# Queries and keys of a head transposed together, copied out whole, split by GpSimd in place and spread over the partitions by four DMAs

## The chip, the cores and the metric

The kernel runs on one core of one Trainium2 chip. The metric is the device time of one execution in microseconds (us), from first to last instruction with a little around it; the profile also gives the span alone.

## What is computed

Three layers in a row: attention in which a query sees only keys of its own cluster, a top-1 mixture of eight experts, and a feed-forward layer. Only the attention is touched by the change.

```python
# q, k, v: (2, 8, 768, 64) float32; centroids: (8, 16, 64)
q_assign = np.argmax(einsum('bhsd,hcd->bhsc', q_n, c_n), axis=-1)   # nearest centroid
k_assign = np.argmax(einsum('bhsd,hcd->bhsc', k_n, c_n), axis=-1)
mask = q_assign[:, :, :, None] == k_assign[:, :, None, :]
scores = np.where(mask, scale * np.matmul(q, k.transpose(0, 1, 3, 2)), -1e9)
attn = softmax(scores);  attn_out = np.matmul(attn, v)
```

## The kernel before

The attention is a loop over 16 (batch, head) pairs, called heads here; the engines' programs are written out by hand and tied by semaphores. A head has six tiles of 128 positions. All big products are made from float32 numbers split in a high part (rounded to the matmul's format, fp32r) and a low part (the rest): a product is high x high plus the cross terms.

Head h is worked on in `attend(h)`, in six steps s = 0..5 on every engine. In a step, TensorE (PE) transposes probabilities (`transpose_probs`, L1245, six transposes), makes the scores of one query tile (`scores`, L1231/L1232, tiles 4 and 5 of head h in s = 0, 1, then tiles 0 to 3 of head h+1), and adds to the output (`prob_values`, L1259/L1261). ScalarE (ACT) copies the transposed probabilities out of PSUM (L629), takes the exponential (`expo`, L603) of the scores whose row maximum VectorE (DVE) has made (`rowmax`, L871); DVE makes the low half of the probabilities (L923). `transpose_probs` at s = 0 and s = 3 waits for the exponentials of three tiles (`exp_done`): at s = 3 the last is that of tile 5, which ACT makes in s = 2. `outputs_back` (L1273, in s = 1 and 4) waits for `o_t`, which ACT copies (L612).

The operands of head h+2 are prepared in between, through one PSUM bank (number 7):

- GpSimd (POOL), `split_operands` (L419, L421): each [128 x 64] tile of q and k becomes [high | low], 128 wide, in `halves`; it runs a head further ahead.
- PE, `operands` (L1185): twelve transposes of `halves` tiles per head, in four batches of three, at s = 0, 2, 3 and 4 (the last one split: one transpose before `outputs_back`, two after). A batch waits for bank 7.
- The batch is copied out by ACT (`copy_operand`, L584) at s = 0, 3 and 4, and by DVE (`copy_second_batch`, L866) at s = 2; queries are scaled by 1/8 on the way.
- `cluster_scores` (L1196, s = 5) multiplies by the centroids, ACT copies `ct_sb` (L598), `cluster_rows` (L1205) brings the scores back to rows, DVE finds the clusters, and in s = 1 of `attend(h+1)` PE transposes their one-hot codes (`onehots`, L1214), which ACT (`copy_onehot`, L592, three copies, in s = 1) and DVE (L859) put beside the operands as extra rows that carry the mask.
- POOL's `copy_queries` (L445) and two DMAs on SP's queue (`move_keys`, L336 then L338, the second after the first has landed) put halves on the other 64 partitions. `scores(h+2, 0)`, in s = 2 of `attend(h+1)`, waits for all of it.

POOL also makes low halves of the first expert's weights in pieces (`split_piece`, L404) in heads 2 to 5 and 8 to 11. At the start the operands of heads 0 and 1 are made outside the loop; `warm` matmuls (L1166) fill PE's waits. At the end of the attention `attend(14)` has no operands to prepare (`ahead` is 1) and `attend(15)` nothing ahead.

In the row names below, `ps` is PSUM, `p_t` the transposed probabilities, `qk_t` the operands of the scores.

Of the kernel before, what the change touches and what calls it, by code (L numbers as in the profile page):

```python
# [26 lines left out]
F32 = mybir.dt.float32  # L27
# [8 lines left out]
P = 128  # L36
# [30 lines left out]
BATCH_OF = {0: 0, 2: 1, 3: 2, 4: 3}  # L67
FIRST_BANKS = ((4, 5, 6, 7), (4, 5, 6, 4))
# [6 lines left out]
WARM = (11, 11, 9)  # L75
# [6 lines left out]
def build(nc, q, k, v, centroids, w_gate, w_ogate, w1, w2, w_in, w_out, out):  # L82
# [58 lines left out]
    raw = place("raw", [P, 2, 2 * QT, D], F32, early)  # L141
    halves = place("halves", [P, 2 * QT, 2 * D], F32R, early)
# [5 lines left out]
    cen_t = place("cen_t", [P, 2, P], F32R, early)  # L148
# [15 lines left out]
    cst = place("cst", [P, 2, 14 * NC], F32R, small)  # L164
# [51 lines left out]
    with ctx:  # L216
# [16 lines left out]
        high_done, halves_done, tr_done, opa_done = sem("high_done"), sem("halves_done"), sem("tr_done"), sem("opa_done")  # L233
        keys_low, keys_high = sem("keys_low"), sem("keys_high")
        b2_done, vs_done, vhi_done = sem("b2_done"), sem("vs_done"), sem("vhi_done")
# [67 lines left out]
        def _(sp):  # L303
            sp.dma_start(cen[:, 0, :], centroids.rearrange("h c d -> (h c) d")).then_inc(cen_in, 16)

            def load_head(h, u):

                if h >= 2:
                    sp.wait_ge(halves_done, 2 * (h - 1))
                sp.dma_start(raw[:, u, 0:QT, :], q_h[bass.ds(h, 1)].squeeze(0)).then_inc(qk_in[u], 16)  # L310
                sp.dma_start(raw[:, u, QT:, :], k_h[bass.ds(h, 1)].squeeze(0)).then_inc(qk_in[u], 16)
# [20 lines left out]
            def move_keys(h):  # L332

                u = h % 2
                sp.wait_ge(ct_done, h + 1)
                sp.dma_start(qk_t[0:D, u, B2:B2 + QT, :].bitcast(F32), qk_t[D:, u, B1:B1 + QT, :].bitcast(F32)).then_inc(keys_low, 16)  # L336
                sp.wait_ge(keys_low, 16 * (h + 1))
                sp.dma_start(qk_t[D:, u, B1:B1 + QT, :].bitcast(F32), qk_t[0:D, u, B1:B1 + QT, :].bitcast(F32)).then_inc(keys_high, 16)  # L338

            move_keys(0)  # L340
            for h in range(2, BH):
                load_head(h, h % 2)
                move_keys(h - 1)
# [5 lines left out]
            move_keys(BH - 1)  # L349
# [14 lines left out]
        def _(pool):  # L364
# [15 lines left out]
            pool.tensor_copy(const_f[:], const_i[:]).then_inc(const_pool, 1)  # L380

# [30 lines left out]
            def split_operands(h, j, i, u, first):  # L412

                if j == 0:
                    pool.wait_ge(qk_in[u], 32 * (i + 1))
                if not first:
                    pool.wait_ge(tr_done, 4 * (h - 1) + 2 * (j + 1))
                t = slice(j * QT, (j + 1) * QT)
                pool.tensor_copy(halves[:, t, 0:D], raw[:, u, t]).then_inc(high_done, 1)  # L419
                pool.wait_ge(high_done, 2 * h + j + 1)  # L420
                pool.tensor_tensor(halves[:, t, D:], raw[:, u, t], halves[:, t, 0:D].bitcast(F32),  # L421
                                   ALU.subtract).then_inc(halves_done, 1)
# [11 lines left out]
            def place_centroids(h, u):  # L434
# [33 lines left out]
            def attend(h, i, u):  # L468
# [11 lines left out]
                if h + 3 < BH:  # L480
                    split_operands(h + 3, 0, i + 1 + u, 1 - u, False)
# [4 lines left out]
                if h + 2 < BH:  # L486
                    copy_queries(h + 2, u)
                if 2 * h < SPREAD:
                    spread(h, 0)
                if h + 3 < BH:  # L490
                    split_operands(h + 3, 1, i + 1 + u, 1 - u, False)
# [3 lines left out]
            split_operands(0, 0, 0, 0, True)  # L495
            split_operands(0, 1, 0, 0, True)
            pool.wait_ge(cen_ev, 2)
            place_centroids(0, 0)
            split_operands(1, 0, 0, 1, False)
            copy_queries(0, 0)  # L500
            split_operands(1, 1, 0, 1, False)
            pool.wait_ge(const_pool, 11)
            candidates(0)
            place_centroids(1, 1)
            split_values(0, 0, 0, True)
            copy_queries(1, 1)
            split_operands(2, 0, 1, 0, False)
            split_operands(2, 1, 1, 0, False)
# [64 lines left out]
        def _(act):  # L573
# [4 lines left out]
            def copy_operand(h, b, u, first, bank=7):  # L578

                if not first and b < 2:  # L580
                    act.wait_ge(s_done, QT * (h - 2) + HALF * (b + 1))
                act.wait_ge(tr_done, 4 * h + b + 1)
                t = (A1, B1)[b // 2] + HALF * (b % 2)
                act.activation(qk_t[:, u, t:t + HALF, :].rearrange("p t n -> p (t n)"), x_bank[bank], ACT.Copy,  # L584
                               scale=QSCALE if b < 2 else 1.0).then_inc(opa_done, 1)
# [28 lines left out]
            def attend(h, u, first, ahead):  # L614
                un = 1 - u
                for s in range(QT):
                    n = QT * h + s
                    if s == 3 and ahead >= 2:
                        copy_operand(h + 2, BATCH_OF[s], u, False)
# [10 lines left out]
                    if s in (0, 4) and ahead >= 2:  # L630
                        copy_operand(h + 2, BATCH_OF[s], u, False)
# [11 lines left out]
            for b in range(4):  # L643
                copy_operand(0, b, 0, True, FIRST_BANKS[0][b])
            copy_cluster_scores(0)
            for b in range(2):
                copy_operand(1, b, 1, True, FIRST_BANKS[1][b])
# [3 lines left out]
            copy_operand(1, 2, 1, True, FIRST_BANKS[1][2])  # L651
            expo(0, 1, 0)
            copy_operand(1, 3, 1, True, FIRST_BANKS[1][3])
# [135 lines left out]
        def _(dve):  # L789
            dve.memset(onehot[:], 0.0)  # L790
            dve.memset(qk_t[D:D + NC, :, A2:A2 + QT, :].bitcast(F32), 0.0)
            dve.memset(cen_s[:, 3, :].bitcast(F32), 0.0)
# [24 lines left out]
            dve.tensor_tensor(cen_s[:, 2, :], cen_u[:], cen_s[:, 0, :].bitcast(F32), ALU.subtract)\  # L817
                .then_inc(cen_d, 1)
            dve.memset(cst[:].bitcast(F32), 0.0).then_inc(cen_ev, 1)
            dve.wait_ge(cen_tr, 1)  # L820
            dve.tensor_copy(cen_t[:].rearrange("p j n -> p (j n)"), ps[:, 6, 0:2 * P]).then_inc(cen_ev, 1)
# [31 lines left out]
            def clusters(h):  # L853
                for step in (highest_score, best_clusters, highest_label, one_hot):
                    step(h)

# [4 lines left out]

            def copy_second_batch(h, u):
                dve.wait_ge(s_done, QT * (h - 2) + 2 * HALF)
                dve.wait_ge(tr_done, 4 * h + 2)
                t = A1 + HALF
# [684 lines left out]
```

## Time and profile before

| | |
|---|---|
| median of 3 runs | 839.55 us (839.29 to 839.87) |
| the profiled execution | 839.41 us |
| its span | 837.6 us |
| mean granted TensorE clock | 0.985 |
| PE busy | 801.6 us (96%) |
| DVE / ACT / POOL busy | 450.6 / 383.2 / 348.0 us |
| DMA queue of SP (q1) | 60.92 MB, 22.5% of 16 engines |

A matmul's end is modelled and matmuls overlap, so the distance between the starts of two rows tells what a group took, not the sum of durations. A row gives start and duration in us, the engine, the line, the operation, what it writes and reads, and in brackets the idle time of the engine before it and what ended that.

### The profile page before, as it was taken

How to read it: one execution, taken by the hardware profiler on the slowest of the kernel's cores; microseconds unless marked ns; L12 is line 12 of the kernel's file. 1: busy time of each engine (PE TensorE's matmuls, PEld its weight loads, DVE VectorE, ACT ScalarE, POOL GpSimd, SP SyncE). 2: the span in 40 equal slices, each digit the busy share in tenths (PEclk: the TensorE clock that was granted, in tenths of full speed). 3: DMA queues.
4: the chain of work that ended last, by engine and by line, in shares of the span. 5: the costliest groups of instructions: out<-in, count | busy, mean ns of one | idle time of the engine just before them, and what ended most of it. 6: DMA issues, size and time to landing. Idle time of an engine off the chain costs nothing.

```text
span 837.6 us, 13745 instructions
## 1 busy us (share of the span) xinstructions
PE 801.6 (96%) x4370; PEld 677.3 (81%) x4371; DVE 450.6 (54%) x795; ACT 383.2 (46%) x757; POOL 348.0 (42%) x343
## 2 busy tenths in 40 slices
PE   7999999999999949999999999989999999999994
PEld 4898999999999727888888888868888888888883
DVE  5788888888888865221221221234455444554442
ACT  4788888888788744222322322212222322332222
POOL 7345654455632028778767767764000100010001
PEclk9999999999999969999999999999999999999998
DMA  4344333423121148699669669682000100010001
GB/s 108 108 123 162 98 116 88 125 57 122 47 61 23 57 154 278 223 336 382 204 241 359 215 241 348 230 287 83 1 1 1 50 1 1 0 51 1 1 0 51
DMA packets 45429, 105.44 MB, mean 126 GB/s; under 512 B 5200, under 2 KB 12880, under 8 KB 44368
## 3 DMA queue, kind: packets, MB, share of 16 engines
q1 hardware_dynamic: 29584, 60.92, 22.5%
q0 software_dynamic: 15808, 44.04, 15.6%
q8 instruction: 21, 0.34, 0.2%
q14 instruction: 16, 0.13, 0.0%
HBM read 92.37 MB, written 6.29 MB: 118 GB/s over the span
## 4 chain that ended last, share of the span: by engine, by line
PE 89%; DVE 3%; ACT 2%; DMA 2%; issue 1%; POOL 1%; DVEq 0%; ACTq 0%; POOLq 0%
PE ps L1493 15%; PE ps L1480 15%; PE ps L1440 13%; PE ps L1420 11%; PE ps L1245 7%; PE ps L1261 4%; PE ps L1231 4%; PE ps L1232 4%; PE ps L1259 4%; PE ps L1273 2%; PE ps L1185 2%; PE ps L1430 2%; DMA raw_w<-in_moe_w 2%; PE ps L1205 2%; PE ps L1196 1%
## 5 line engine op out<-in xcount | busy, mean ns | idle before, releaser
L394 POOL TENSOR_TENSOR weights<-raw_w,weights 128x2048 fp32r<-128x2048 f32 x34 | 157.1, 4622 | 49.2 <-DMA weights<-in_moe_w 35.3
L1493 PE MATMUL ps<-weights,g_t 128*128 128x512 f32 x576 | 141.2, 394 | 2.5 <-DVE g_t L1151 2.5
L1480 PE MATMUL ps<-y_t,weights 128*128 128x512 f32 x576 | 139.3, 391 | 0.0
L1493 PEld LDWEIGHTS ps<-weights,g_t 128*128 128x128 f32 x576 | 107.3, 188 | 27.3 <-DVE g_t L1151 4.1
L1480 PEld LDWEIGHTS ps<-y_t,weights 128*128 128x128 f32 x576 | 108.1, 188 | 23.8
L923 DVE TENSOR_TENSOR p_t<-ps,p_t 128x384 fp32r<-128x384 f32 x192 | 98.9, 550 | 27.4 <-ACT p_t L629 27.0
L1420 PE MATMUL ps<-weights,x_t 128*128 x456 | 111.1, 399 | 1.7 <-DVE x_t L1084 1.7
L1440 PE MATMUL ps<-weights,h_t 128*128 x456 | 109.6, 396 | 2.3 <-issue 1.7
L565 POOL DMA_INDIRECT out<-y_sb,order_u x12 | 11.8, 979 | 240.3 <-ACT y_sb L776 238.4
L760 ACT ACTIVATE ps<-g_a,half 128x512 f32<-128x512 f32 x48 | 33.2, 692 | 149.7 <-DVE g_b L1146 149.7
L1420 PEld LDWEIGHTS ps<-weights,x_t 128*128 128x128 f32 x456 | 85.2, 190 | 20.0 <-issue 2.4
L1440 PEld LDWEIGHTS ps<-weights,h_t 128*128 128x128 f32 x456 | 84.3, 188 | 20.3 <-issue 2.8
L629 ACT ACTIVATE p_t<-ps 128x384 fp32r<-128x384 f32 x192 | 83.7, 490 | 24.4 <-PE ps L1245 24.0
L871 DVE TENSOR_REDUCE nmax<-ps 128x1 f32<-128x768 f32 x96 | 91.0, 949 | 4.9 <-PE ps L1232 3.3
L603 ACT ACTIVATE prob<-ps,nmax 128x768 f32<-128x768 f32 x96 | 87.2, 908 | 1.3 <-DVE nmax L871 0.9
L1245 PE MATMUL ps<-ident,prob 128*128 128x128 f32 x576 | 79.2, 273 | 1.3 <-ACT prob L603 0.8
L1231 PE MATMUL ps<-qk_t 128*128 128x384 f32 x192 | 73.2, 381 | 1.1 <-ACT prob L603 1.1
L1245 PEld LDWEIGHTS ps<-ident,prob 128*128 128x128 f32 x576 | 66.4, 140 | 5.0 <-ACT prob L603 1.8
L1261 PE MATMUL ps<-p_t,v_s 128*128 128x384 f32 x192 | 67.1, 350 | 1.1 <-DVE x_sb L897 0.6
L1232 PE MATMUL ps<-qk_t 80*128 80x384 f32 x192 | 65.1, 339 | 0.0
L714 ACT ACTIVATE h_t<-ps 128x1024 fp32r<-128x1024 f32 x19 | 19.5, 1025 | 92.3 <-PE ps L1430 92.3
L1145 DVE TENSOR_SCALAR g_a<-ps 128x512 f32<-128x512 f32 x48 | 33.1, 689 | 49.7 <-PE ps L1480 49.6
(178 smaller groups left out, 1076.4 us busy)
## 6 DMA issues: line engine op xcount, KB each, us to landing
raw_w<-in_moe_w SPq DMA_DIRECT2D x32, 1024.0 KB, 6.2
weights<-in_moe_w POOLq DMA_DIRECT2D x28, 1024.0 KB, 9.1
qk_t<-qk_t SPq DMA_DIRECT2D x32, 192.0 KB, 2.6
raw_w<-in_moe_w_in SPq DMA_DIRECT2D x4, 1024.0 KB, 6.0
weights<-in_moe_w_in POOLq DMA_DIRECT2D x4, 1024.0 KB, 7.8
raw_w<-in_moe_w_out SPq DMA_DIRECT2D x4, 1024.0 KB, 7.9
weights<-in_moe_w_out POOLq DMA_DIRECT2D x4, 1024.0 KB, 12.7
raw<-in_q SPq DMA_DIRECT2D x16, 192.0 KB, 2.9
```

The lines of the kernel that those rows point to most:

```text
L394: pool.tensor_tensor(weights[:, unit % 2, 1, c * CHUNK:(c + 1) * CHUNK], low_chunk(unit, c), high_chunk(unit, c).bitcast(F32), ALU.subtrac ...
L603: act.activation(prob[:, c, :].rearrange("p (a n) -> p a n", a=2), s_ps[c % 2], ACT.Exp, bias=nmax[:, c % 2:c % 2 + 1], accum_out=sums[:, ...
L871: dve.tensor_reduce(nmax[:, c % 2:c % 2 + 1], s_ps[c % 2], AX.XY, ALU.max, negate=True)\
L923: dve.tensor_tensor(p_t[:, s % 2, 1, t], pt_ps[:, t], p_t[:, s % 2, 0, t].bitcast(F32), ALU.subtract).then_inc(ptl_done, 1)
L1231: mm(o, qk_t[:, u, A1 + c, :], b1, start=True, stop=False)
L1232: last = mm(o, qk_t[0:D + NC, u, A2 + c, :], b2, start=False, stop=True)
L1245: last = tr(ps[:, 4 + t, c * P:(c + 1) * P], prob[:, HALF * g + c, k:k + P], ident[:])
L1261: last = mm(ot_ps, v_s[:, u, k, :], p_t[:, s % 2, 0, t, :], start=(k == 0), stop=(k == QT - 1))
L1420: last = mm(ps[:, n, :], x_t[:, u, a, k, :], flat[:, bass.ds(base + (b * UNIT + w), BANK)], start=(k == 0 and j == 0), stop=(k == KC - 1 a ...
L1440: last = mm(ps[:, 5 + u, :], h_t[:, a, n, :], flat[:, bass.ds(base + (b * UNIT + w), DM)], start=(n == 0 and j == 0), stop=(n == FC - 1 an ...
L1480: last = mm(ps[:, 4 + n % 2, :], wi[:, a, k, f * P:(f + 1) * P], y_ts[g % 2][:, b, k, :], start=(k == 0 and j == 0), stop=(k == KC - 1 and ...
L1493: last = mm(ps[:, t, :], g_t[:, n % 2, a, t * P:(t + 1) * P], wo[:, b, f, :], start=(f == 0 and j == 0), stop=(f == FC2 - 1 and j == 2))
```

## The change

`raw` holds q and k of a tile side by side, [128 x (64 | 64)], loaded so by the two DMAs (runs of 64 numbers instead of 384). PE transposes it unsplit: six transposes per head in two batches, at s = 0 and s = 2. The result, queries on partitions 0 to 63 and keys on 64 to 127, is copied out whole by ACT (`copy_whole`) with a scale per partition (1/8 or 1, the new tile `qscale`). POOL makes the high and the low half from that copy in place in `qk_t` (`split_operands`, after the transposes now). Four DMAs per head place the halves on the other partitions (`place_halves`). DVE's copy at s = 2 and POOL's `copy_queries` are gone, ACT's copies at s = 3 and 4 too, one at s = 2 is new. `copy_onehot` also waits for `k_low`. The centroids' table `cen_t` and `cst` are laid out for the new order (as many matmuls as before). At the start ACT makes the high half and DVE the low half out of PSUM, and the `warm` counts differ.

```diff
-BATCH_OF = {0: 0, 2: 1, 3: 2, 4: 3}
+BATCH_AT = {0: 0, 2: 1}
-WARM = (11, 11, 9)
+WARM = (5, 3, 11, 9)
...
# SP
-                    sp.wait_ge(halves_done, 2 * (h - 1))
-                sp.dma_start(raw[:, u, 0:QT, :], q_h[...])...
-                sp.dma_start(raw[:, u, QT:, :], k_h[...])...
+                    sp.wait_ge(tr_done, 2 * (h - 1))
+                sp.dma_start(raw[:, u, :, 0:D], q_h[...])...
+                sp.dma_start(raw[:, u, :, D:], k_h[...])...
...
+            def place_halves(h):
+                sp.wait_ge(high_done, 2 * (h + 1))
+                sp.dma_start(qk_t[0:D, u, A1:A1 + 2 * QT, :]..., high[0:D]...broadcast_to([D, 2, QT, P])).then_inc(q_high, 16)
+                sp.wait_ge(low_done, 2 * (h + 1))
+                sp.dma_start(qk_t[D:, u, A1:A1 + QT, :]..., low[0:D]).then_inc(q_low, 16)
                 sp.wait_ge(ct_done, h + 1)
+                sp.wait_ge(q_low, 16 * (h + 1))
+                sp.dma_start(low[0:D], low[D:]).then_inc(k_low, 16)
+                sp.wait_ge(q_high, 16 * (h + 1))
+                sp.dma_start(high[0:D], high[D:]).then_inc(k_high, 16)
...
# POOL
+            def split_operands(h, b, u):
+                if b == 0:
+                    pool.wait_ge(s_done, QT * (h - 1))
+                pool.wait_ge(whole_done, 2 * (h - 2) + b + 1)
+                pool.tensor_copy(hi, whole[:, b]).then_inc(high_done, 1)
+                pool.wait_ge(high_done, 2 * h + b + 1)
+                pool.tensor_tensor(lo, whole[:, b], hi.bitcast(F32), ALU.subtract).then_inc(low_done, 1)
...
# ACT
+            def copy_whole(h, b):
+                act.wait_ge(low_done, 2 * (h - 1) + b + 1)
+                act.wait_ge(tr_done, 2 * h + b + 1)
+                act.activation(whole[:, b], x_ps, ACT.Copy, scale=qscale[:, 0:1]).then_inc(whole_done, 1)
 
             def copy_onehot(h, j, u):
                 act.wait_ge(oh_tr, h + 1)
+                act.wait_ge(k_low, 16 * (h + 1))
...
-                    if s == 3 and ahead >= 2:
-                        copy_operand(h + 2, BATCH_OF[s], u, False)
+                    if s == 2 and ahead >= 2:
+                        copy_whole(h + 2, BATCH_AT[s])
...
# DVE
-                    if s == 2 and ahead >= 2:
-                        copy_second_batch(h + 2, u)
...
# PE
+                if b == 0:
+                    pe.wait_ge(qk_in[u], 32 * (i + 1))
+                for n in range(HALF):
+                    last = tr(x_bank[bank][:, n * P:(n + 1) * P], raw[:, u, HALF * b + n, :], ident[:])
...
-                    if s in (2, 3) and ahead >= 2:
-                        operands(h + 2, BATCH_OF[s], ...)
+                        operands(h + 2, BATCH_AT[s], i + 1, u, (oh_done, 2 * h + 4))
...
                     if s == 4:
-                        if ahead >= 2:
-                            operands(h + 2, 3, (opa_done, 4 * h + 11), (0,))
                         outputs_back(2 * h, h, u, first)
-                        if ahead >= 2:
-                            operands(h + 2, 3, None, (1, 2))
```

How ACT's instructions stood before, inside the loop, from the exponential of step 1 to the copy out of bank 7 in step 3:

```order
L603 ACTIVATE prob,sums<-ps,nmax 128x768 [waits max_done]
L626 ISA
L629 ACTIVATE p_t<-ps 128x384 [waits pv_done,pt_done]
L626 REGISTER_ALU
L629 ACTIVATE p_t<-ps 128x384 [waits pt_done]
L602 REGISTER_ALU
L603 ACTIVATE prob,sums<-ps,nmax 128x768 [waits max_done]
L582 REGISTER_ALU
L584 ACTIVATE qk_t<-ps 128x384 [waits tr_done]
```

How they stand there now, from the exponential of step 1 to that of step 2:

```order
L600 ACTIVATE prob,sums<-ps,nmax 128x768 [waits max_done]
L579 REGISTER_ALU
L580 REGISTER_ALU [waits low_done]
L581 ACTIVATE whole<-ps,qscale 128x384 [waits tr_done]
L623 ISA
L626 ACTIVATE p_t<-ps 128x384 [waits pv_done,pt_done]
L623 REGISTER_ALU
L626 ACTIVATE p_t<-ps 128x384 [waits pt_done]
L599 REGISTER_ALU
L600 ACTIVATE prob,sums<-ps,nmax 128x768 [waits max_done]
```

The copy out of bank 7 stood behind the exponential of step 2; now it stands ahead of that step's probabilities and exponential.

PE at the start of step 3 before, with the batch of that step:

```order
L1183 REGISTER_ALU [waits halves_done]
L1185 MATMUL ps<-ident,halves 128x128 [waits opa_done]
L1185 MATMUL ps<-ident,halves 128x128 x2
L1238 REGISTER_ALU
L1242 ISA [waits exp_done]
L1245 MATMUL ps<-ident,prob 128x128 [waits ptl_done]
```

And now, from the last two products of step 2:

```order
L1263 MATMUL ps<-p_t,v_s 64x384 [waits ptl_done]
L1265 MATMUL ps<-p_t,v_s 128x384
L1242 REGISTER_ALU
L1246 ISA [waits exp_done]
L1249 MATMUL ps<-ident,prob 128x128 [waits ptl_done]
```

Nothing stands between the last product of step 2 and the wait for the exponentials any more.

## Rows read from the trace of the kernel before

**Rows 1.** The page, part 2: granted TensorE clock in 40 slices of the span.
```profile
PEclk9999999999999969999999999999999999999998
```
**Rows 2.** Timeline of PE: the first and 14th cluster scores in the loop; between them `attend(7)`.
```profile
37.80 0.86 PE L1196 MATMUL ps<-qk_t,cst 128*128 128x384 f32 x4
...
145.76 0.82 PE L1245 MATMUL ps<-ident,prob 128*128 128x128 f32 x6
...
153.91 0.49 PE L1185 MATMUL ps<-ident,halves 128*128 128x128 f32 x3
...
154.23 0.82 PE L1245 MATMUL ps<-ident,prob 128*128 128x128 f32 x6
...
156.96 0.27 PE L1185 MATMUL ps<-ident,halves 128*128 128x128 f32 x1
...
157.78 0.38 PE L1185 MATMUL ps<-ident,halves 128*128 128x128 f32 x2
157.91 0.42 PE L1231 MATMUL ps<-qk_t 128*128 128x384 f32 x1
...
159.40 0.86 PE L1196 MATMUL ps<-qk_t,cst 128*128 128x384 f32 x4
...
163.02 0.82 PE L1245 MATMUL ps<-ident,prob 128*128 128x128 f32 x6
...
263.65 0.87 PE L1196 MATMUL ps<-qk_t,cst 128*128 128x384 f32 x4
```
**Rows 3.** Timeline of ACT in the same head, steps 0 to 2.
```profile
146.36 0.87 ACT L629 ACTIVATE p_t<-ps 128x384 fp32r<-128x384 f32 x2 [1.20 <-PE ps L1245]
147.12 0.50 ACT L584 ACTIVATE qk_t<-ps 128x384 fp32r<-128x384 f32 x1
147.49 0.91 ACT L603 ACTIVATE prob<-ps,nmax 128x768 f32<-128x768 f32 x1
...
148.94 0.48 ACT L592 ACTIVATE qk_t<-ps 16x384 fp32r<-16x384 f32 x1
...
152.29 0.87 ACT L629 ACTIVATE p_t<-ps 128x384 fp32r<-128x384 f32 x2
...
153.83 0.21 ACT L603 ACTIVATION_READ_ACCUMULATOR prob<-ps,nmax 128x1 f32 x1
```
**Rows 4.** Timeline of ACT, PE and its weight load in `attend(14)`, steps 2 to 5.
```profile
274.86 0.22 ACT L603 ACTIVATION_READ_ACCUMULATOR prob<-ps,nmax 128x1 f32 x1
...
275.13 0.64 PEld L1245 LDWEIGHTS ps<-ident,prob 128*128 128x128 f32 x6 [0.22 <-ACT prob L603]
...
278.70 0.42 PE L1231 MATMUL ps<-qk_t 128*128 128x384 f32 x1
```
**Rows 5.** ACT's copies by line: duration ns min/median/max; L668 has a scale per partition.
```profile
L629 ACT ACTIVATE p_t<-ps x192: 480/490/501, 24.8 to 295.9; 128x384 fp32r<-128x384 f32 x192
L714 ACT ACTIVATE h_t<-ps x19: 1007/1026/1027, 328.5 to 548.0; 128x1024 fp32r<-128x1024 f32 x19
L668 ACT ACTIVATE x_sb<-ps,rsum x3: 305/313/313, 299.5 to 299.9; 128x64 f32<-128x64 f32 x3
```
**Rows 6.** Timeline of `attend(2)`, step 4: DVE's reciprocals and PE's wait.
```profile
69.21 1.16 DVE L876 TENSOR_SCALAR rsum<-sums 128x6 f32<-128x6 f32 x1
...
72.11 0.44 PE L1261 MATMUL ps<-p_t,v_s 128*128 128x384 f32 x1 [0.31 <-DVE normal L897]
```
**Rows 7.** Timeline of the first 25 us: DVE, SP's queue, PE.
```profile
6.44 1.04 DVE L817 TENSOR_TENSOR cen_s<-cen_u,cen_s 128x64 fp32r<-128x64 f32 x1
...
5.55 1.67 SPq L320 DMA_DIRECT2D gates<-in_moe_w_output_gate  x2
...
17.02 0.53 PE L1231 MATMUL ps<-qk_t 128*128 128x384 f32 x1
...
24.25 0.88 PE L1245 MATMUL ps<-ident,prob 128*128 128x128 f32 x6
```
**Rows 8.** The first of the two key DMAs (L336, 192 KB within SBUF), 16 times.
```profile
DMA to landing us min/median/max: 2.5/2.5/3.9
```

More of the change, by code:

```diff
@@ L66 @@
 OHW = P
[L67 to L68 removed]
+BATCH_AT = {0: 0, 2: 1}
+FIRST_BANKS = ((4, 5), (6, 4))
 SPREAD = 2 * (BH - 2)
@@ L140, in build @@
     early = [slot1]
-    raw = place("raw", [P, 2, 2 * QT, D], F32, early)
-    halves = place("halves", [P, 2 * QT, 2 * D], F32R, early)
+    raw = place("raw", [P, 2, QT, 2 * D], F32, early)
+    whole = place("whole", [P, 2, GW], F32, early)
+    qscale = place("qscale", [P, 1], F32, early)
     v_sb = place("v_sb", [P, 2, QT, D], F32, early)
@@ L576, in _, with first_high @@
             act.activation(cen_n[:, 1:2], cen_n[:, 0:1], ACT.Sqrt).then_inc(cen_a, 1)
[L578 to L585, printed above, removed]
+            def first_high(h, b, bank):
+                act.wait_ge(tr_done, 2 * h + b + 1)
+                t = B1 + HALF * b
+                act.activation(qk_t[:, h, t:t + HALF, :].rearrange("p t n -> p (t n)"), x_bank[bank], ACT.Copy,
+                               scale=qscale[:, 0:1]).then_inc(high_done, 1)
+            def copy_whole(h, b):
+                act.wait_ge(low_done, 2 * (h - 1) + b + 1)
+                act.wait_ge(tr_done, 2 * h + b + 1)
+                act.activation(whole[:, b], x_ps, ACT.Copy, scale=qscale[:, 0:1]).then_inc(whole_done, 1)
             def copy_onehot(h, j, u):
                 act.wait_ge(oh_tr, h + 1)
+                act.wait_ge(k_low, 16 * (h + 1))
                 for t, row, scale, bias in ((A2, 64 * j, -1.0, 1.0), (B2, 64 * j + 32, -MASKED, 0.0))[1 - j:]:
@@ L629, in attend @@
                         act.activation(p_t[:, s % 2, 0, t], pt_ps[:, t], ACT.Copy).then_inc(pth_done, 1)
-                    if s in (0, 4) and ahead >= 2:
-                        copy_operand(h + 2, BATCH_OF[s], u, False)
+                    if s == 0 and ahead >= 2:
+                        copy_whole(h + 2, BATCH_AT[s])
                     if s == 1 and ahead >= 1:
@@ L1166, in warm, with operands @@
                     mm(ps[:, IDLE_BANK, :], ones[:], ones[:].unsqueeze(1).broadcast_to([P, BANK // P, P]), start=True, stop=True)
+            def operands(h, b, i, u, free, bank=7):
+                if b == 0:
+                    pe.wait_ge(qk_in[u], 32 * (i + 1))
+                if free:
+                    pe.wait_ge(*free)
+                for n in range(HALF):
+                    last = tr(x_bank[bank][:, n * P:(n + 1) * P], raw[:, u, HALF * b + n, :], ident[:])
+                last.then_inc(tr_done, 1)
             pe.wait_ge(const_pool, 11)
             warm(WARM[0])
+            for b in range(2):
+                operands(0, b, 0, 0, None, bank=FIRST_BANKS[0][b])
+            warm(WARM[1])
             pe.wait_ge(cen_d, 11)
@@ L1174, in _ @@
             last.then_inc(cen_tr, 1)
-            def operands(h, b, free, tiles=range(HALF), bank=7):
-                if b % 2 == 0:
-                    pe.wait_ge(halves_done, 2 * h + b // 2 + 1)
-                if free:
-                    pe.wait_ge(*free)
-                for n in tiles:
-                    last = tr(x_bank[bank][:, n * P:(n + 1) * P], halves[:, HALF * b + n, :].bitcast(F32), ident[:])
-                if HALF - 1 in tiles:
-                    last.then_inc(tr_done, 1)
             def cluster_scores(h, u):
-                pe.wait_ge(opa_done, 4 * h + 4)
+                pe.wait_ge(low_done, 2 * (h + 1))
                 pe.wait_ge(cst_done, h + 1)
-                for n, t in enumerate((A1, B1, A1 + HALF, B1 + HALF)):
-                    cols = slice(2 * NC * (3 - n), 2 * NC * (3 - n) + P)
-                    last = mm(ct_ps, cst[:, u, cols], qk_t[:, u, t:t + HALF, :].rearrange("p t n -> p (t n)"),
-                              start=(n == 0), stop=(n == 3))
+                for a in range(2):
+                    cols = slice(4 * NC * (1 - a), 4 * NC * (1 - a) + P)
+                    for t in (B1, B2):
+                        last = mm(ct_ps, cst[:, u, cols],
+                                  qk_t[:, u, t + a * HALF:t + (a + 1) * HALF, :].rearrange("p t n -> p (t n)"),
+                                  start=(a == 0 and t == B1), stop=(a == 1 and t == B2))
                 last.then_inc(ct_done, 1)
@@ L1221, in scores @@
                     pe.wait_ge(ohq_done, h + 1)
-                    pe.wait_ge(b2_done, h + 1)
-                    pe.wait_ge(keys_high, 16 * (h + 1))
+                    for moved in (q_high, q_low, k_low, k_high):
+                        pe.wait_ge(moved, 16 * (h + 1))
                 if not (first and c < 2):
@@ L1275, in outputs_back, with attend @@
                 last.then_inc(back_done, 1)
-            def attend(h, u, first, ahead):
+            def attend(h, i, u, first, ahead):
                 un = 1 - u
```

141 lines of the change are left out of this document (60 added, 81 removed).

## The prediction

> **What bounds the kernel now.** I read the page's slices first: the granted clock is full over the attention, the first 13 slices [rows 1], so times there can be taken as they stand. Then PE's timeline of one head [rows 2]. The starts of step 0 of two heads are 163.02 - 145.76 = 17.26 us apart, and PE runs through with no idle time marked. So work taken off PE looks like time gained. The timeline of ACT for the same head [rows 3] says otherwise: its steps 0 to 2 are one unbroken chain. From the first copy of the probabilities at 146.36 it runs to the end of the accumulator read at 153.83 + 0.21 = 154.04, when the exponential of tile 5 is released. PE's transposes of step 3, which wait for it, start at 154.23 [rows 2]. How soon PE can follow is seen in `attend(14)`, which has no operand batches: the read ends at 274.86 + 0.22 = 275.08, PE's weight load starts at 275.13 and is marked as having waited for it [rows 4]. That is 0.05 us; in a normal head there are 0.19, so ACT has only 0.14 us to spare per head in this half of the loop. A head is thus bound twice: steps 0 to 2 almost equally by PE and ACT, steps 3 to 5 by PE alone.
>
> **The change, part by part.**
>
> *PE's six transposes less per head.* The batch of step 3 took 154.23 - 153.91 = 0.32 us; of step 4's, the first tile took some 0.11 (the batch of step 3 shows 0.32 / 3) and the last two 157.91 - 157.78 = 0.13 [rows 2]. That is 0.56 us per head, the whole gross gain, over 14 heads (0 to 13) 7.8 us. What of it reaches the end depends on what PE meets next.
>
> *ACT's copy in step 2.* Before, DVE copied the batch of step 2; now ACT does, ahead of that step's probabilities and of the exponential that step 3 waits for. Copies of 384 elements take 490 ns, and the next instruction starts 0.37 us after such a one (147.12 to 147.49) [rows 5, 3]. But `copy_whole` scales per partition. The nearest row for that is the copy at L668, 64 elements in 313 ns. The two copies without it give (1026 - 490) / 640 = 0.84 ns per element [rows 5], so 64 elements would take 490 - 320 x 0.84 = 221 ns: the scale per partition adds 0.09 us. I take 0.37 + 0.09 = 0.46 us for the copy in step 2, and 0.09 for the one in step 0, which was there before without it. The bounds are 0.37 in all (the scale free) and 0.58 + 0.09 (no overlap with the next instruction). Sum taken: 0.55 us more on the chain. 0.14 is spare, so the transposes of step 3 start 0.41 us later than before, and the 0.32 us that PE had won there is a wait.
>
> The Trainium skill ("ScalarE: Activation LUTs", section "What ACT_TABLE_LOAD costs") speaks against this change: each pointer operand of an activation adds about 93 ns, and back-to-back activations overlap by about 93 ns. By it the copy is 599 ns, some 506 on the chain, and an estimate with it gives 0.34 us more per head in place of the 0.29 below, so 840.9 us in place of 840.2. The rows agree on the 0.09.
>
> *Steps 3 to 5.* `attend(14)` shows this stretch without batches: from the transposes' weight load at 275.13 to the scores of step 4 at 278.70 it takes 3.57 us, against 157.91 - 154.23 = 3.68 in a normal head [rows 4, 2]. So of 0.24 us taken off step 4, 0.11 arrive: `outputs_back` has to wait for `o_t`, and that wait was filled by the transpose at 156.96. I take 0.12. ACT's removed copies in steps 3 and 4 are worth nothing: ACT waits for PE there. Net per head +0.41 - 0.12 = +0.29 us, 14 x 0.29 = **+4.1 us**.
>
> *POOL.* `copy_queries` goes; the four splits now follow the copy of step 2, which ends some 0.9 us before step 3 begins, and end some 2 us later; the cluster scores that wait for `low_done` are 5 us further on (159.40) [rows 2], so the splits cost nothing, unless a weight piece delays them; these stand behind. Where POOL works, DVE's tiny L876 is held (1.16 us in `attend(2)`) and PE ends up waiting for the normalised outputs, marked 0.31 [rows 6]. The 14 cluster scores from 37.80 to 263.65 are 225.85 us apart [rows 2]; 13 undisturbed heads would be 13 x 17.27 = 224.5. These 1.3 us come from heads in which the splits were late for the load of k or pieces and `copy_queries` ran long. Now the loads have a head of slack and `copy_queries` is gone, but the pieces end about as late. I take **-1.0 us** (0 to -1.3).
>
> *DVE's* copy in step 2 is hidden, it lies beside ACT's chain: nothing.
>
> *SP's queue.* Four DMAs per head for two. The new series is `low_done` to `q_low` to `k_low`, and `ct_done` to `k_low`. `k_low` can be issued when the cluster scores end, 160.3, and ACT's one-hot copy needs it where 148.94 stands a head earlier, 166.20 [rows 2, 3]. That leaves 5.9 us for a landing of 2.5, at most 3.9 [rows 8]: nothing. Before, the two key DMAs ran one after the other, now side by side.
>
> *The start.* From 0 to 24.25, where the loop's first transposes start [rows 7], everything is a chain. It loses POOL's splits ahead of the transposes, and DVE's centroid steps no longer run beside them: L817 took 1.04 us for 64 columns [rows 7] where such a step takes some 0.2. I estimate the first low halves at about 8.0. SP is held by its nine loads: the gates' end at 5.55 + 1.67 = 7.22 [rows 7], and q and k in short runs should add about a microsecond. So `q_low`, behind `q_high`, goes out at about 8.8, lands at 11.3 with the 2.5 of [rows 8], `k_low` lands at 13.9, and three one-hot copies of 0.49 lead to the first scores at 15.5 against 17.02 [rows 7]: 1.5 us earlier. Between the first exponentials two copies of 0.37 go (0.8 us with their waits). I take **-2.3 us**; bounds 0 (loads and DMAs in series give all back) and -2.9 (the DMAs don't bind). After the attention nothing is changed, and everything there waits for it.
>
> **Sum** against the profiled execution: 839.4 + 4.1 - 1.0 - 2.3 = **840.2 us**. That execution is 0.14 us from the median of the runs, 839.55; no shift is made. A measurement of this kernel tells about 0.2%, 1.7 us, from no change, so this is within it (837.9 to 841.2).
>
> **The rivals.**
>
> - *ACT's scale is free* (0.17): the copy costs 0.37 on the chain and nothing in step 0. Net 0.37 - 0.14 - 0.12 = 0.11 per head, 1.5 us: 837.6. For it: the pitch of 0.37 in [rows 3]. Against: L668 [rows 5].
> - *PE stays the bound* (0.08): if the exponential of tile 5 was not what step 3 meets, PE's 0.56 us per head arrive: 839.4 - 7.8 - 1.0 - 2.3 = 828.3. Against it: in `attend(14)` PE waits for ACT even with ACT a copy shorter [rows 4].
> - *The copy doesn't overlap* (0.15), the slower side: 0.58 + 0.09 - 0.14 = 0.53 at step 3, and step 4 gives nothing: 14 x 0.53 = 7.4, 843.5. It decides as soon as the copy in step 2 takes over 0.55 us of ACT's chain. For it: more waits stand ahead of the new copy.
> - *The start gives nothing* (0.15): SP's longer issue and the series of DMAs eat it: 842.5.
> - *`k_low` becomes the wait* (0.05): where a weight load of 1 MB is on the queues the landing exceeds 5.9 us. ACT, and PE behind it, would lose some 2 us in each of five heads: 850. Against: the longest landing of 3.9 [rows 8].
> - The forecast has 0.40, its own range 838.5 to 842.
>
> **How the numbers follow.** The likeliest is 840.2. The range of 836.8 to 843.8 takes in the free scale, the copy without overlap and the start without gain, and leaves out PE as the bound, the late DMA and tails. Faster than 837.9: PE as the bound 0.08, most of the free scale 0.11, the forecast's tail 0.04, together 0.23. Slower than 841.2: 0.15 + 0.05 + 0.12 of the start and 0.05 of the forecast's tail, 0.37. Within: 0.40.
>
> **What would show it.** In a normal head, PE's transposes of step 3 are marked as waiting for the exponential, and heads are 17.5 to 17.6 us apart; `copy_whole` lasts 0.58; in step 4 PE waits for `o_t`. The loop's first transposes start near 22. L876 still shows long durations in the heads with pieces. I am wrong if heads get shorter than 17.26 (then PE was the bound), if ACT's one-hot copies wait for a DMA, or if the first transposes stay near 24.

## The result and the profile after

The changed kernel takes **842.38 us** (median of 6 runs, 842.20 to 844.15), the kernel before, run beside it, 839.67 (839.29 to 841.99, 6 runs). The ratio is 1.0035, 95% interval [1.0025, 1.0045]. That is 0.35% slower, by more than the 0.2% that such a measurement can tell. The prediction had 840.2, a range of 836.8 to 843.8, and 0.37 for this side: the time lies in the range; the likeliest case, no change, did not come. The profiled execution took 842.27 us (span 840.5), 2.86 more than that of the kernel before.

First the page of the kernel before, from parts 4 and 5:

```profile
PE 89%; DVE 3%; ACT 2%; DMA 2%; issue 1%; POOL 1%; DVEq 0%; ACTq 0%; POOLq 0%
...
L1245 PE MATMUL ps<-ident,prob 128*128 128x128 f32 x576 | 79.2, 273 | 1.3 <-ACT prob L603 0.8
```

And of the changed kernel, parts 2, 4 and 5:

```profile
PEclk9999999999999978999999999999999999999998
...
PE 79%; ACT 11%; issue 5%; DVE 3%; DMA 1%; ACTq 0%; POOL 0%; SPq 0%; DVEq 0%
...
L1249 PE MATMUL ps<-ident,prob 128*128 128x128 f32 x576 | 79.8, 274 | 8.3 <-ACT prob L600 7.9
```

The clock over the attention is full, as in [rows 1]. ACT's share of the chain that ended last was 2% and is now 11%. PE's transposes of the probabilities, L1245 before and L1249 now, waited 0.8 us for exponentials and now wait 7.9. The timeline of PE says where. It shows `attend(7)`, and the first and the last cluster scores of the loop, for [rows 2]:

```profile
37.31 0.85 PE L1199 MATMUL ps<-qk_t,cst 128*128 128x384 f32 x4
...
146.77 0.82 PE L1249 MATMUL ps<-ident,prob 128*128 128x128 f32 x6
...
155.65 0.87 PE L1249 MATMUL ps<-ident,prob 128*128 128x128 f32 x6 [0.53 <-ACT prob L600]
...
158.49 0.90 PE L1277 MATMUL ps<-back_w,o_t 128*128 128x80 f32 x6
159.18 0.42 PE L1235 MATMUL ps<-qk_t 128*128 128x384 f32 x1
...
159.79 0.33 PE L1236 MATMUL ps<-qk_t 80*128 80x384 f32 x1
160.05 0.44 PE L1265 MATMUL ps<-p_t,v_s 128*128 128x384 f32 x1
...
160.84 0.85 PE L1199 MATMUL ps<-qk_t,cst 128*128 128x384 f32 x4
...
267.04 0.34 PE L1199 MATMUL ps<-qk_t,cst 128*128 128x384 f32 x1
```

From step 0 to step 3 a head takes 155.65 - 146.77 = 8.88 us; it took 154.23 - 145.76 = 8.47 [rows 2]. From step 3 to step 5's cluster scores it takes 5.19, before 5.17. The 14 cluster scores from 37.31 to 267.04 are 229.73 us apart, where they were 225.85: +3.88 us in 13 heads. The first two are 17.38 apart (before 17.27), all others evenly 17.67 to 17.72; the 1.3 us of stalls are gone. At the start 37.31 stands for 37.80, -0.49. Together that is +3.39 when the last of them starts. The rest, up to the end of the span, takes 573.46 us where it took 573.95.

ACT's timeline, steps 0 to 2 and the beginning of 3, answers to [rows 3]:

```profile
147.37 0.87 ACT L626 ACTIVATE p_t<-ps 128x384 fp32r<-128x384 f32 x2 [1.17 <-PE ps L1249]
148.13 0.59 ACT L581 ACTIVATE whole<-ps,qscale 128x384 f32<-128x384 f32 x1
...
149.47 0.51 ACT L609 ACTIVATE o_t<-ps 128x384 f32<-128x384 f32 x1
...
153.30 0.57 ACT L581 ACTIVATE whole<-ps,qscale 128x384 f32<-128x384 f32 x1
153.77 0.87 ACT L626 ACTIVATE p_t<-ps 128x384 fp32r<-128x384 f32 x2
...
155.30 0.22 ACT L600 ACTIVATION_READ_ACCUMULATOR prob<-ps,nmax 128x1 f32 x1
156.23 0.87 ACT L626 ACTIVATE p_t<-ps 128x384 fp32r<-128x384 f32 x2 [0.71 <-PE ps L1249]
```

The chain is unbroken from 147.37 to 155.52, `copy_whole` takes 0.57 to 0.59 us, the next instruction starts 0.46 to 0.47 after its start, and PE starts 0.13 after the end of the chain. The start, PE and SP's queue, for [rows 7]:

```profile
5.91 1.54 PE L1175 MATMUL ps<-ident,raw 128*128 128x128 f32 x6 [0.59 <-DMA raw<-in_k]
7.25 1.42 PE L1166 MATMUL ps<-ones 128*128 128x512 bf16 x3
8.50 0.38 PE L1185 MATMUL ps<-ident,cen_s 128*128 128x128 f32 x2
10.48 0.96 PE L1199 MATMUL ps<-qk_t,cst 128*128 128x384 f32 x4 [1.60 <-DVE qk_t L790]
17.35 0.53 PE L1235 MATMUL ps<-qk_t 128*128 128x384 f32 x1
23.62 0.87 PE L1249 MATMUL ps<-ident,prob 128*128 128x128 f32 x6
...
8.10 0.72 SPq L339 DMA_DIRECT2D qk_t<-qk_t  x1
10.46 0.51 SPq L342 DMA_DIRECT2D qk_t<-qk_t  x1
13.15 0.48 SPq L345 DMA_DIRECT2D qk_t<-qk_t  x1
```

The first scores came 0.33 us later than before, not 1.5 earlier, the loop's first transposes 0.63 earlier.

### The profile page after: what moved, and what is told of

Same layout as the page of the kernel before. It is cut to its first block, busy times and chain, and to the rows that moved or that the text cites. A ratio compares the mean times of both kernels' runs of the same rounds, so it can differ in the third digit from the quotient of the medians.

```text
span 840.5 us, 13536 instructions
## 1 busy us (share of the span) xinstructions
PE 796.6 (95%) x4271; PEld 666.3 (79%) x4272; DVE 442.8 (53%) x786; ACT 378.1 (45%) x739; POOL 331.8 (39%) x321
## 4 chain that ended last, share of the span: by engine, by line
PE 79%; ACT 11%; issue 5%; DVE 3%; DMA 1%; ACTq 0%; POOL 0%; SPq 0%; DVEq 0%
PE ps L1487 15%; PE ps L1474 15%; PE ps L1414 13%; PE ps L1434 12%; PE ps L1249 5%; ACT prob L600 5%; ACT p_t L626 3%; PE ps L1265 2%; PE ps L1235 2%; PE ps L1236 2%; ACT qk_t L589 2%; PE ps L1263 2%; PE ps L1424 2%; PE ps L1277 2%; PE ps L1209 2%
## 5 line engine op out<-in xcount | busy, mean ns | idle before, releaser
L1249 PE MATMUL ps<-ident,prob 128*128 128x128 f32 x576 | 79.8, 274 | 8.3 <-ACT prob L600 7.9
L1249 PEld LDWEIGHTS ps<-ident,prob 128*128 128x128 f32 x576 | 66.2, 140 | 16.3 <-DVE p_t L918 11.2
L1265 PE MATMUL ps<-p_t,v_s 128*128 128x384 f32 x192 | 67.6, 352 | 0.7 <-DVE x_sb L894 0.6
```

The costliest lines, as they stand in the source:

```text
L1249: last = tr(ps[:, 4 + t, c * P:(c + 1) * P], prob[:, HALF * g + c, k:k + P], ident[:])
L1265: last = mm(ot_ps, v_s[:, u, k, :], p_t[:, s % 2, 0, t, :], start=(k == 0), stop=(k == QT - 1))
```

## The experiments

Twelve kernels, each beside runs of the kernel before. Ratios are to it.

**1. The copy of step 2 back on VectorE** (`dve_second`), all else as changed.

```diff
@@ ScalarE
-                    if s == 2 and ahead >= 2:
-                        copy_whole(h + 2, BATCH_AT[s])
@@ VectorE
+                dve.tensor_scalar(whole[:, b], x_ps, qscale[:, 0:1], None, ALU.mult).then_inc(whole_done, 1)
...
+                    if s == 2 and ahead >= 2:
+                        copy_whole(h + 2, BATCH_AT[s])
```

> The changed kernel with one edit: the copy out of bank 7 in step 2 is made by DVE, in the place in which DVE made it before the change. My theory: this copy lengthens ACT's unbroken chain of steps 0 to 2, and PE's transposes of step 3 wait for it (heads 17.68 us apart against 17.27). Then the stretch from step 0 to step 3 falls from 8.88 to about 8.42 (0.60 to ACT's first copy, 7.68 of chain, 0.09 for the scale, 0.05 to PE), the heads to 17.2, the whole by 14 x 0.46 to about 836. Rival A: the loop is longer because of the new waits, the DMAs or POOL's splits; then it stays at 842. Rival B: DVE's copy pushes DVE's low halves and it gains only half, 839.

Measured: 837.11 us (11 runs), 0.9977 [0.9968, 0.9987], faster than both kernels. VectorE's and ScalarE's timelines of step 2:

```profile
150.23 0.61 DVE L867 TENSOR_SCALAR whole<-ps,qscale 128x384 f32<-128x384 f32 x1
...
152.03 0.21 ACT L600 ACTIVATION_READ_ACCUMULATOR prob<-ps,nmax 128x1 f32 x1
```

PE's transposes of step 0 start at 143.90 and those of step 3 at 152.37, 8.47 us as in the kernel before; heads are 17.30 apart. The theory had 8.42, 17.2 and about 836 us: PE starts 0.13 us after ScalarE's chain, not 0.05, and steps 3 to 5 take 5.23 for 5.19. The copy is hidden on VectorE; on ScalarE it is what made the change slower.

**2. Both copies on VectorE** (`dve_both`): the same for step 0, where VectorE copies ahead of its low halves of the probabilities.

> Both copies of a head out of bank 7 are made by DVE, at step 0 and step 2. My theory: ACT's chain loses another 0.46 us, so that PE, not ACT, ends the stretch from step 0 to step 3: 8.47 less the batch of step 3 (0.32) is 8.15; with 5.2 and 3.6 for the rest a head takes 16.95, 14 x 0.73 less than the changed kernel, about 832. Rival: DVE's own chain at the turn from step 0 to step 1 (low halves, row maximum, one-hot copy, normalisation) becomes the wait; then it is no better than with the second copy alone on DVE, about 836.

Measured: 840.20 us (11 runs), 1.0010 [1.0001, 1.0019], so worse than one copy. ScalarE in step 0 of `attend(7)`, and VectorE in step 0 of `attend(6)`, by their timelines:

```profile
148.26 0.49 ACT L609 ACTIVATE o_t<-ps 128x384 f32<-128x384 f32 x1 [0.32 <-PE ps L1268]
...
129.54 0.62 DVE L865 TENSOR_SCALAR whole<-ps,qscale 128x384 f32<-128x384 f32 x1 [0.27 <-issue]
```

Without its copy ScalarE waits 0.32 us for PE's products before `o_t`: the copy of step 0 lay mostly in a gap, and steps 0 to 3 take 8.47 us in such a head, as with one copy. But in the heads with which a new round of the loop begins (it holds two heads), `attend(4)`, `attend(6)` and on to `attend(12)`, VectorE stands idle for about 0.3 us ahead of the copy. The profile names nothing for it but "issue", and PE's transposes for it had ended at 129.08 in the head shown. The low halves behind the copy come later, and the head takes 17.7 us (124.31 to 141.99); the others, after the first, take 17.28 to 17.43. The rival had named VectorE's chain at this turn, but with 836 us; why the idle time arises was not tried.

**3. ScalarE's copy one exponential later** (`act_late`): ahead of step 3's work instead of step 2's, still on ScalarE.

```diff
-                    if s == 2 and ahead >= 2:
-                        copy_whole(h + 2, BATCH_AT[s])
+                    if s == 3 and ahead >= 2:
+                        copy_whole(h + 2, 1)
```

> The changed kernel with ACT's copy of step 2 moved behind that step's exponential, to the head of step 3 where ACT copied before the change. ACT does exactly as much. My theory (order on ACT's chain counts, not its load): the exponential is released 0.46 us sooner, as with DVE's copy, about 836. Rival: ACT's load as such, or the new DMAs, set the pace: 842. POOL's splits start 1.6 us later and still end ahead of the cluster scores; if they don't, in the heads with weight pieces, PE waits at step 5 and part of the gain is lost.

Measured: 841.54 us (5 runs), 1.0036 [1.0022, 1.0049]. Heads without weight pieces are 17.26 to 17.30 apart, as expected; those with pieces, 17.88 to 17.96. POOL, VectorE and PE of such a head, by the timeline:

```profile
102.92 1.01 POOL L431 TENSOR_TENSOR qk_t<-whole,qk_t 128x384 fp32r<-128x384 f32 x1
103.90 2.52 POOL L415 TENSOR_TENSOR weights<-raw_w,weights 128x512 fp32r<-128x512 f32 x2
...
103.97 1.22 DVE L873 TENSOR_SCALAR rsum<-sums 128x6 f32<-128x6 f32 x1
...
106.95 0.44 PE L1265 MATMUL ps<-p_t,v_s 128*128 128x384 f32 x1 [0.53 <-DVE normal L894]
```

The splits end 1.5 us later than in the changed kernel, so the weight piece runs beside VectorE's instruction on the six sums (L873), which takes 1.22 us for 0.34 in the changed kernel's same head, and PE waits 0.53 us for the normalisation. Eight such heads at 0.6 us each are the 4.8 us that lie between this result and some 836.7, near the theory's 836; the other heads show what the theory said. The forecast had named late splits in these heads, but with another wait, that of the cluster scores in step 5. The time of a copy is not only its own engine's matter, it also sets when POOL disturbs VectorE.

**4. The scale as a constant** (`scale_const`): `scale=1.0` for `scale=qscale[:, 0:1]` in `copy_whole`. It leaves the factor of 1/8 on the queries out.

> The changed kernel with a constant scale of 1 in copy_whole in place of the scale per partition; it leaves out the queries' factor of 1/8 in heads 2 to 15. My theory: the scale per partition costs 0.09 us for each of two copies on ACT's chain, so 14 x 0.18 = 2.5 us less, 839.8. Rival: the scale is free, 842.3.

Measured: 841.23 us (10 runs), 1.0024 [1.0015, 1.0034]. Between the theory (839.8) and its rival (842.3). ScalarE's timeline:

```profile
130.77 0.50 ACT L581 ACTIVATE whole<-ps 128x384 f32<-128x384 f32 x1
131.14 0.92 ACT L600 ACTIVATE prob<-ps,nmax 128x768 f32<-128x768 f32 x1
```

The exponential now starts 0.37 us after the start of the copy, where it was 0.46: the scale per partition is 0.09 us for each copy. Heads take 17.53 and 17.59 in turn, 17.56 for 17.70, and steps 0 to 3 take 8.75 for 8.88. So 0.13 of the 0.18 us arrives: the copy of step 2 is on the chain in full, and that of step 0 falls for the most part into the gap of experiment 2.

**5. PE's six transposes put back** (`spare_tr`), into a PSUM bank that nobody reads then.

```diff
+                    if s == 3 and ahead >= 2:
+                        pe.wait_ge(whole_done, 2 * h + 2)
+                        spare(u, (0, 1, 2))
...
+                            spare(u, (0,))
                         outputs_back(2 * h, h, u, first)
+                            spare(u, (1, 2))
```

> The changed kernel with six transposes of TensorE put back per head, three in step 3 and three in step 4, where the kernel before had its third and fourth batch; they write a PSUM bank that nobody reads. Theory (ScalarE sets steps 0 to 3, and what is taken off PE in step 4 is given back to the wait for the normalised outputs): the three in step 3 lie in the 0.53 us that PE waits for the exponential there, so step 0 to step 3 stays at 8.88; step 3 to step 5 stays within 0.1 us of 5.19. 842 to 843.5 us. Rival (PE's time counts): 0.56 us in each of 14 heads, 7.8 us more, 850 us, heads 18.3 us apart.

Measured: 844.04 us (6 runs, 841.69 to 844.99), 1.0047 [1.0032, 1.0062]. In the head, the theory holds to 0.03 us:

```profile
148.70 0.82 PE L1253 MATMUL ps<-ident,prob 128*128 128x128 f32 x6
...
156.90 0.49 PE L1193 MATMUL ps<-ident,raw 128*128 128x128 f32 x3
157.58 0.87 PE L1253 MATMUL ps<-ident,prob 128*128 128x128 f32 x6 [0.19 <-ACT prob L600]
```

8.88 us to step 3 with and without them, and heads 17.70 apart. So what PE was spared is worth nothing after the change, and the rival (850 us, heads 18.3) is out. The median is 0.5 us above the theory's 842 to 843.5. The profiled execution, one of the upper ones with 844.16, lost time at the start: the granted clock there fell (below), and the first cluster scores of the loop came at 39.00 instead of 37.31. Whether the other upper ones did so too, no profile shows.

**6. The centroids' transposes ahead of three warm-up matmuls** (`cen_first`).

```diff
-            warm(WARM[1])
             pe.wait_ge(cen_d, 11)
...
             last.then_inc(cen_tr, 1)
+            warm(WARM[1])
```

> The changed kernel with the centroids' two transposes ahead of the second group of three warm-up matmuls at the start. Theory (the start gained only 0.6 us of the predicted 2.3 because PE's queue, warm-up first, holds the centroids' transposes, their copies and then the low halves until 10.48): the first cluster scores start 1 us earlier, near 9.5, the loop's first transposes near 22.6, and the time is 841.4. Rival (the DMAs of the operands, which start when SP is through its loads, bind the first scores): the cluster scores come earlier but the first scores stay at 17.35, 842.3. Heads unchanged at 17.7 in both.

Measured: 842.49 us (6 runs, 842.23 to 846.51), 1.0046 [1.0029, 1.0062]: the rival. PE, SP's queue and ScalarE, by the timeline:

```profile
17.23 0.44 PE L1235 MATMUL ps<-qk_t 128*128 128x384 f32 x1 [0.87 <-ACT qk_t L589]
...
8.07 0.63 SPq L339 DMA_DIRECT2D qk_t<-qk_t  x1
9.10 0.51 SPq L342 DMA_DIRECT2D qk_t<-qk_t  x1
13.07 0.48 SPq L345 DMA_DIRECT2D qk_t<-qk_t  x1
...
15.70 1.48 ACT L589 ACTIVATE qk_t<-ps 16x384 fp32r<-16x384 f32 x3 [4.13 <-DMA qk_t<-qk_t]
```

The cluster scores came 1.35 us earlier (9.13), the first scores 0.12. `q_low`, L342, went out 1.36 us earlier and landed 3.9 us later instead of 2.6, behind the 384 KB of `q_high`; `k_low`, which waits for it, went out at 13.07 for 13.15.

**7. The kernel before with its copy of step 2 on ScalarE** (`old_act_second`).

```diff
-                    if s == 3 and ahead >= 2:
+                    if s in (2, 3) and ahead >= 2:
                         copy_operand(h + 2, BATCH_OF[s], u, False)
```

> The kernel before with one thing altered: the copy of the operands' second batch, in step 2, goes from VectorE to ScalarE. PE's work, POOL's splits and the DMAs stay as they were. Theory (the place of this copy on ScalarE is what costs the change its time): the copy takes 0.37 us of the chain, 0.14 were spare, so heads are 0.23 us longer, 17.5 us apart, and the time is 839.5 + 14 x 0.23 = 842.7 us. Rival (PE sets the head in the kernel before, ScalarE has room): 839.5 us, heads 17.27 apart.

Measured: 842.45 us (6 runs), 1.0040 [1.0027, 1.0053]. Heads are 17.58 apart. The rival is out, and this one edit costs about all that the whole change costs. The step from 0 to 3 grew by 0.26 (8.73), the rest by 0.05.

**8. Experiments 1 and 6 together** (`second_cen`).

> The changed kernel with both repairs: the copy in step 2 on VectorE, and the centroids' transposes ahead of the warm-up. Theory: heads 17.30 us apart as with the first repair alone (837.1 us, 0.9977 of before), and the start 1 us earlier: 836 us, 0.9965. Rival (the operands' DMAs bind the start): 837.1, no gain from the second repair.

Measured: 837.25 us (11 runs), 0.9977 [0.9968, 0.9985]: the rival again, nothing from the second.

**9. The outputs of step 4 in a PSUM bank of their own** (`back_bank`). The matmuls of values and probabilities (L1265) write the bank from which VectorE normalises; the new order leaves bank 7 free there. PE's wait for the normalisation moves from these matmuls to the cluster scores of step 5, which use bank 7 too.

```diff
-        back_ps = ps[:, 6, 0:HALF * BACK].rearrange(...)
+        back_of = [ps[:, 7 - g, 0:HALF * BACK].rearrange(...) for g in range(2)]
...
+                        pe.wait_ge(norm_done, 2 * h + 1)
                         cluster_scores(h + 2, u)
```

> The changed kernel with the transposed-back outputs of step 4 written to PSUM bank 7, which the new order leaves free in steps 3 and 4, instead of bank 6, into which the next matmuls of probabilities and values go. Theory (the 0.12 us that step 4 should have given after the change is eaten by the wait of those matmuls for VectorE's normalisation, which the two transposes behind outputs_back used to cover): with the wait gone, step 3 to step 5 falls from 5.19 to 5.07 us, heads to 17.55, and 14 x 0.12 = 1.7 us are gained: 840.7. Rival (the stretch is bound by ScalarE's o_t and the probabilities' copies, the wait only fills a gap): 5.19 stays, 842.4.

Measured: 840.97 us (11 runs), 1.0013 [1.0004, 1.0022]. Rows of PE's timeline:

```profile
156.10 0.87 PE L1250 MATMUL ps<-ident,prob 128*128 128x128 f32 x6 [0.52 <-ACT prob L601]
...
160.25 0.34 PE L1237 MATMUL ps<-qk_t 80*128 80x384 f32 x1
160.43 0.33 PE L1266 MATMUL ps<-p_t,v_s 128*128 128x384 f32 x1
...
161.12 0.68 PE L1200 MATMUL ps<-qk_t,cst 128*128 128x384 f32 x3
```

161.12 - 156.10 = 5.02 us for 5.19, heads 17.53 to 17.58, as the theory had it. The scores' last matmul and L1266 are 0.18 us apart, where 159.79 and 160.05 were 0.26: the normalisation did hold PE there, though no idle time is marked.

**10. `q_low` ahead of `q_high` in the first head** (`low_first`), on top of experiment 8.

```diff
+                if not late:
+                    place_high()
                 sp.wait_ge(low_done, 2 * (h + 1))
                 sp.dma_start(qk_t[D:, u, A1:A1 + QT, :].bitcast(F32), low[0:D]).then_inc(q_low, 16)
+                if late:
+                    place_high()
```

> The kernel with both repairs (copy of step 2 on VectorE, centroids first) and, for the first head alone, the DMA of the queries' low halves issued ahead of that of their high halves. With the centroids first the low DMA took 3.9 us to land behind the high one, 2.6 without that haste. Theory (it is held by the high one's traffic): the keys' low DMA goes out near 11.8 instead of 13.1, the first scores start near 16.2, 836.2 us. Rival (all four DMAs together bind the first scores, whichever goes first: now the keys' high halves, behind the queries' high ones, come last): first scores at 17.1 or later, 837.2 or up to 1 us more.

Measured: 836.39 us (6 runs), 0.9962 [0.9950, 0.9974]. Between the theories: `k_low` went out at 11.81 as expected, but the first scores, at 16.82, then waited 0.47 us for a DMA: 0.3 us earlier than in experiment 8 (17.14), where 0.9 was hoped for. In the totals the gain is within the intervals.

**11. and 12. The combinations**: experiments 1, 6 and 9 (`three`), and with 10 as well (`all_four`).

> The changed kernel with the copy of step 2 on VectorE, the centroids' transposes first and the outputs of step 4 in bank 7. Theory: each repair gives what it gives alone, heads of 17.30 - 0.12 = 17.18 us, 837.2 - 1.7 = 835.5 us, 0.9955 of before. Rival (step 3 to step 5 bound elsewhere): 837.2, as without the bank.

> The changed kernel with all four repairs: the copy of step 2 on VectorE, the centroids' transposes first, the queries' low DMA of the first head first, and the outputs of step 4 in bank 7. Theory: they add up. Heads 17.15 us apart, first scores at 16.8: 836.7 - 0.35 = 836.3 us, 0.996 of before. Rival (the free PSUM bank and the earlier start only move the wait, as the loads of the next head's q and k go out later): heads back at 17.3 or first scores at 17.2, 837 us or more.

Measured: 836.70 us (5 runs), 0.9964 [0.9951, 0.9978], and 836.09 (6 runs), 0.9962 [0.9947, 0.9976]. Heads are 17.12 to 17.16 us apart in both, so the two repairs of the loop add up, as the theories said (17.18 and 17.15). The total of `three` does not decide: 836.70 lies between the theory's 835.5 and the rival's 837.2, and the interval holds both. `all_four` came as expected (836.3, first scores at 16.75). The intervals of the three fastest versions (`low_first`, `three`, `all_four`) overlap; which is best is not settled, but each is faster than both kernels, by less than 1%.

## Why the prediction was right or wrong

The mechanism in the first half of a head was right. Two terms failed, the gain in steps 3 to 5 and the start, and that the time still fell into the range says little for them.

- **ScalarE sets steps 0 to 3: right, and the 0.41 us exact, by luck: two errors cancel.** I summed 0.55 us more on the chain less 0.14 to spare. The chain from step 0's transposes to the end of the read went from 154.04 - 145.76 = 8.28 to 155.52 - 146.77 = 8.75, by 0.47. From the start of `o_t` to the end, where the copy of step 2 lies, it grew by 0.44 (6.05 for 5.61); of step 0's 0.09 some 0.03 arrived (`o_t` starts 2.70 us after step 0's transposes, where it was 148.43 - 145.76 = 2.67). And only 0.06 were to spare, since PE starts 0.13 after the end, not 0.05; the 0.05 of [rows 4] is the weight load's. Experiments 1 and 7 show the mechanism from both sides.
- **The scale per partition: right.** 0.09 us for each copy by experiment 4. The Trainium skill ("ScalarE: Activation LUTs", section "What ACT_TABLE_LOAD costs") has about 93 ns for each pointer operand, and the trace agrees with that: 0.46 us from copy to exponential with it, 0.37 without. The rival of a free scale is out.
- **Steps 3 to 5 give -0.12: the step that failed in the loop.** Measured +0.02. I read 3.57 us from `attend(14)` for the stretch to the scores of step 4, and it came: 159.18 - 155.65 = 3.53, against 3.68. But I ended the reading there. Behind the scores PE waits for VectorE's normalisation, which starts when `outputs_back` is through. VectorE and PE by the timeline, before and, below, after:

```profile
158.07 0.41 DVE L897 TENSOR_TENSOR normal<-ps,rsum 128x240 f32<-128x240 f32 x1 [0.33 <-PE ps L1273]
158.70 0.34 PE L1261 MATMUL ps<-p_t,v_s 128*128 128x384 f32 x1
```
```profile
159.51 0.41 DVE L894 TENSOR_TENSOR normal<-ps,rsum 128x240 f32<-128x240 f32 x1 [0.35 <-PE ps L1277]
```

  Before, the normalisation ended at 158.48, 0.22 us before PE's matmul: the two transposes that stood between had covered it. Now it ends at 159.92, and PE's matmul starts 0.13 behind it, at 160.05. 14 x 0.14 = 2.0 us too little. Experiment 9, which takes the shared bank away, gets 0.17 us in this stretch, and in experiment 5 the transposes fit in again for 0.03.
- **Stalls -1.0: right in kind**, measured -1.3, the bound. The long durations on the six sums in heads with pieces, which I expected to stay, are gone (0.34 to 0.36 us now, up to 1.16 before), and experiment 3, where they are back, shows how such stalls arise.
- **The start -2.3: the other failed term**, measured -0.63: the first transposes at 23.62, where I had named 22 as the sign of being right and 24 of being wrong. Of its parts, -0.8 between the exponentials came (-0.96); -1.5 for the first scores became +0.33. I had the low halves at 8.0 and `q_low` out at 8.8; it went at 10.46. The operand transposes waited for the short-run load of k until 5.91, the warm-up took 1.42 us behind them, and the centroids' transposes, whose input was ready at 6.00, stood behind that in PE's queue until 8.50. But this order alone is not what costs. In experiment 6 the cluster scores came 1.35 us earlier and the first scores only 0.12; in experiment 10 they waited for a DMA. So, freed of the order, the start is bound by the four DMAs, 960 KB together, of which I had priced each by itself.
- **The other rivals:** PE as the bound is refuted by experiment 5, the late `k_low` by the profile (no wait in the loop), the copy without overlap by the 0.46 us from its start to the next instruction's. "The start gives nothing" (842.5) came nearest, with 0.15, but by chance: the start gave 0.63, and 2.0 us of the time are the gain in steps 3 to 5 that did not come.

By its terms: 14 x (0.41 + 0.02) = +6.0 for +4.1, -1.3 for -1.0, -0.6 for -2.3. The sum would be 843.5. The first two heads took less: from the loop's first transposes to its first cluster scores 13.69 us for 13.55, and the next head 17.38 for 17.27, so +0.25 for the two in place of +0.86; why they grew less was not tried. And from the last cluster scores to the end it took 0.49 less, for which I had nothing. With these the sum is 842.4, for 842.27 in the profiled execution. The 0.49 need no cause of their own: that stretch took 573.0 to 574.3 us in 13 of the 14 profiles, and its code is nearly the same in all.

## What to carry to other kernels

When work is taken off an engine that runs without gaps, look for the chain that runs just as long beside it: 0.06 us of slack decided over 0.56 us of saved matmuls here, and a small copy that changes engines can cost more than the saving. Follow a shortened stretch to the next instruction that is shared by two engines, past the wait that you know: what stood in between may have been a cover. Price transfers that are issued together as a group, not one by one.

## What the runs showed of the hardware

- **The granted clock at the start is not the same in every execution.** Here are stretches of 4 us, PE's windows of two kernels (us, PE busy, PEclk, DMA share, GB/s), `back_bank` and `spare_tr`:

```profile
20.00:24.00 4.00, 3.79 (x13) 0.57 0.22 48
24.00:28.00 4.00, 3.45 (x26) 1.00 1.03 201
```
```profile
20.00:24.00 4.00, 3.38 (x11) 0.60 0.39 83
```

  It was 0.57 to 0.60 from 20 to 24 us in four profiles (`scale_const`, `spare_tr`, `back_bank`, `all_four`) and 1.00 in the other ten. The two levels are 1.2 and 2.4 GHz, so PE was at the lower one for most of the stretch. It had been idle for about 1.4 us before, waiting for the first exponential, in all profiles of the changed kernel and its variants, whether the clock fell or not (0.71 in the kernel before). Where it fell, four cluster-score matmuls took 1.49 us for 0.86, and some 1.3 us were lost by the end of the first head. Why it falls in some executions is open. It is a part of the spread of 2 to 3 us that these kernels show, but not all: in the profile of `dve_second`, which took 838.73 us where the median was 837.11, the clock at the start was full, and the stretch behind the last cluster scores took 575.64 us for 573.0 to 574.3 in the others. So compare heads as well as totals.
- **The first matmuls are slow at a granted clock of 1.00.** In the changed kernel three warm-up matmuls at 7.25 us took 1.42 us, six of them at 16.24 took 1.46, and the profile has 1.00 for both stretches. Why is open.
- **A DMA's landing depends on what was issued just ahead.** `q_low`, 192 KB within SBUF, landed in 2.6 us when it was issued 2.4 us behind `q_high`, in 3.9 when 1.0 us behind. Over all heads the median is 3.8; in the loop it goes out about 1.1 us behind (48.52 and 49.61).
